# A chunked linear-attention and two-MLP kernel: one mask copied by another engine, two steps of round 2 put off, the waits of merged slots moved forward

## What is computed

```
for t in range(S):
    cur = np.einsum('bhd,bhe->bhde', u[None] * kt, vt)
    y[:, :, t] = np.einsum('bhd,bhde->bhe', rt, state + cur)
    state = wt[:, :, :, None] * state + np.einsum('bhd,bhe->bhde', kt, vt)
...
a = x @ w_a; b = x @ w_b                       # 384 x 1536
x = a * b @ w_out                              # 1536 x 384
h = x @ w_in                                   # 384 x 2048
g = np.maximum(h, 0.0) + alpha * np.minimum(h, 0.0)
out = g @ w_out                                # 2048 x 384
```

## Time and profile before

| | |
|---|---|
| median of 3 runs | 1011.1 us (1010.41 to 1011.45) |
| profiled execution, its time | 1010.97 us |
| its span, first to last instruction | 1009.2 us |
| mean granted TensorE clock | 0.998 |
| TensorE busy | 987.4 us (98%) |
| VectorE busy | 586.3 us (58%) |
| ScalarE busy | 296.8 us (29%) |
| GpSimd busy | 24.1 us (2%), all of it in the first 47 us |

### The profile page before, as it was taken

How to read it: one execution, slowest core, us unless ns; L and a number is a source line. 1 busy time by engine, 2 the same in 40 slices (tenths; PEclk the granted TensorE clock), 3 DMA queues, 4 the chain that set the end, 5 groups by cost and what they waited for, 6 DMA issues and landing times.

```text
span 1009.2 us, 26702 instructions
## 1 busy us (share of the span) xinstructions
PE 987.4 (98%) x11200; PEld 963.8 (96%) x11200; DVE 586.3 (58%) x1209; ACT 296.8 (29%) x628; POOL 24.1 (2%) x24
## 2 busy tenths in 40 slices
PE   5799999999999999999999999999999999999998
PEld 5799999999999999999999999999999999999998
DVE  7796765855857658567432437555555555555554
ACT  3435314223242242341223324222222222222212
POOL 4400000000000000000000000000000000000000
PEclk9999999999999999999999999999999999999999
DMA  6554311312113013110020414010101010101000
GB/s 174 144 149 121 93 38 34 111 30 65 53 29 92 25 36 87 53 37 2 25 60 15 128 32 126 8 40 11 38 13 35 13 34 14 32 16 32 20 6 23
DMA packets 42126, 52.88 MB, mean 52 GB/s; under 512 B 5152, under 2 KB 42016, under 8 KB 42016
## 3 DMA queue, kind: packets, MB, share of 16 engines
q1 hardware_dynamic: 40624, 51.04, 17.7%
q10 hardware_dynamic: 1392, 0.25, 0.2%
HBM read 39.48 MB, written 9.44 MB: 48 GB/s over the span
## 4 chain that ended last, share of the span: by engine, by line
PE 95%; DVE 3%; issue 1%; ACT 0%; ACTq 0%; DMA 0%; DVEq 0%; SPq 0%
PE products L170 18%; PE products L172 16%; PE products L171 16%; PE acc L170 12%; PE acc L171 12%; PE acc L172 12%; PE products L740 3%; PE products L758 1%; PE products L800 1%; PE products L816 1%; PE products L715 1%; PE products L785 1%; PE products L772 1%; DVE f_y L986 1%; DVE k_in L998 1%
## 5 line engine op out<-in xcount | busy, mean ns | idle before, releaser
L170 PE MATMUL products<-x_parts,weights_hi 128*128 128x384 f32 x576 | 202.2, 351 | 2.6 <-DMA x_parts<-f_y 2.0
L172 PE MATMUL products<-x_parts,weights_lo 128*128 128x384 f32 x576 | 195.1, 339 | 0.3 <-issue 0.3
L171 PE MATMUL products<-x_parts,weights_hi 128*128 128x384 f32 x576 | 194.7, 338 | 0.0
L1375 DVE TENSOR_SCALAR leaky_low<-products,leaky_al 128x384 f32<-128x384 f32 x128 | 79.1, 618 | 169.9 <-PE products L172 169.8
L1322 ACT ACTIVATE leaky_g_hi<-leaky_g_sb 128x384 fp32r<-128x384 f32 x128 | 67.3, 526 | 295.5 <-DVE leaky_g_sb L1380 183.8
L1235 DVE TENSOR_TENSOR g_sb<-a_g,products 128x384 f32<-128x384 f32 x96 | 53.1, 553 | 158.9 <-issue 90.8
L549 ACT ACTIVATE g_hi<-g_sb 128x384 fp32r<-128x384 f32 x96 | 50.3, 524 | 254.5 <-DVE g_sb L1235 254.5
L170 PEld LDWEIGHTS products<-x_parts,weights_hi 128*128 128x128 f32 x576 | 108.0, 187 | 7.8 <-issue 2.7
L172 PEld LDWEIGHTS products<-x_parts,weights_lo 128*128 128x128 f32 x576 | 108.2, 188 | 0.7 <-issue 0.7
L171 PEld LDWEIGHTS products<-x_parts,weights_hi 128*128 128x128 f32 x576 | 108.2, 188 | 0.0
L170 PE MATMUL acc<-g_hi,weights_hi 128*128 128x384 f32 x288 | 96.6, 336 | 0.0
(11 more groups left out here) (94 smaller groups left out, 1757.4 us busy)
## 6 DMA issues: line engine op xcount, KB each, us to landing
k_in<-in_k_dram SPq DMA_DIRECT2D x16, 336.0 KB, 3.9
r_in<-in_r_dram SPq DMA_DIRECT2D x16, 336.0 KB, 5.2
stage<-in_w_out_dram SPq DMA_DIRECT2D x14, 384.0 KB, 3.3
w_v<-in_v_dram SPq DMA_DIRECT2D x16, 288.0 KB, 3.6
y_dram<-x_in SPq DMA_DIRECT2D x8, 576.0 KB, 4.6
x_in<-y_dram SPq DMA_DIRECT2D x8, 576.0 KB, 4.6
out_dram<-leaky_out_sb SPq DMA_DIRECT2D x7, 576.0 KB, 3.3
stage<-in_w_dram SPq DMA_DIRECT2D x10, 336.0 KB, 3.8
```

What stands on the lines that cost most here:

```text
L170: pe.matmul(out, w_hi, x_hi, start=first, stop=False)
L171: pe.matmul(out, w_hi, x_lo, start=False, stop=False)
L172: return pe.matmul(out, w_lo, x_hi, start=False, stop=last)
L1375: dve.tensor_scalar(self.low[f % 2][:, :], h, 0.0, self.al[:, f:f + 1], ALU.min, ALU.mult).then_inc(self.low_ready, 1)
```

## The change

Three things. `copy_four_mask` goes from VectorE (phase 7 of round 0) to ScalarE, behind its preparation of k and r, ahead of the first split of weights. In round 2 the first steps of stream 1 leave phase 0: that of r (`step_r(n, 1, 0)`) comes at the end of phase 1, that of k (`first_step_k(n, 1)`) in phase 2 between the merge of stream 0 and the planes of stream 1. And the five waits of a merged slot stand ahead of the last third of `up_b` of the same block, in all of rounds 2 to 7, in phases 2 and 3; ahead of the slot only the wait for `g_ready` stays.

```diff
+                def copy_four_mask():
+
+                    act.wait_ge(masks_loaded, 32)
+                    dims = [2 * FOUR, Q // (2 * FOUR)]
+                    copy(view(four_mask, 0, [dims, [FOUR, 2], [1, FOUR]], P),
+                         view(level_mask, 0, [dims, [0, 2], [1, FOUR]], P)).then_inc(four_mask_ready, 1)
...
                 act.dma_start(ident[:, :], constants[0:ROWS, 0:ROWS]).then_inc(ident_loaded, 16)
+                copy_four_mask()
                 for step in range(BEFORE_TILES):
...
-                def four(n, j, g):
+                def wait_four(n, j):
 
                     pe.wait_ge(merged, merges(n, 0, 3))
                     pe.wait_ge(fours_merged, fours(n, j))
                     pe.wait_ge(k_first[j], n + 1)
                     pe.wait_ge(fours_copied[j], fours_round(n))
                     pe.wait_ge(fours_stepped[j], 2 * fours_round(n))
+
+                def four(n, j, g):
+
...
                         if kt == KT - 1 and f == F1 - 1 and tile < TILES - 1:
                             for block in range(KT):
                                 wait_x(tile + 1, block)
+                        if kt == KT - 1 and step_at(g) is not None:
+                            n, phase = divmod(step_at(g), PHASES)
+                            if n >= FOURS_FROM and phase in (2, 3):
+                                wait_four(n, phase - 2)
                         product = up_part(g, "w_b", b_ps(g), kt)
...
-                def first_steps(n):
-
-                    for j in range(2):
-                        first_step_k(n, j)
-                        step_r(n, j, 0)
+                def first_steps(n, j):
+
+                    first_step_k(n, j)
+                    step_r(n, j, 0)
...
                         if n == 2:
-                            first_steps(n)
+                            first_steps(n, 0)
...
                         if n == 1:
-                            first_steps(n)
+                            first_steps(n, 0)
+                            first_steps(n, 1)
                         products_of_w(n, 0, 2 if n < FOURS_FROM else 1, range(1, 7))
                         if n >= FOURS_FROM:
                             prepare_fours(n, 0)
+                        if n == 2:
+                            step_r(n, 1, 0)
                     elif phase == 2 and n >= FOURS_FROM:
                         merge_fours(n, 0)
+                        if n == 2:
+                            first_step_k(n, 1)
                         prepare_fours(n, 1)
...
-                    elif phase == 7 and n == 0:
-                        copy_four_mask()
-                    elif phase == 7:
+                    elif phase == 7 and n > 0:
```

More of the change, by code:

```diff
@@ L1021, in merge_level @@
                                         view(products, level_bank(phase, 0), [[BANK, 2], [32, 2 * CH], [h, 32 // h], [1, h]], P)).then_inc(merged, 2)
[L1023 to L1028, removed]
                 def prepare_fours(n, j):
```

## The result

The changed kernel took 1027.5 us, median of 5 (1026.3 to 1028.4), beside 1011.1 us before: 1.0161 times as long, 95% interval 1.0146 to 1.0176. Slower by 16.4 us, on the side that was forecast, and outside the range of 1020.0 to 1024.2.

The account below looks back on a forecast made before the run. It took TensorE, holding 95% of the chain, as the bound. Mask -2.0, round 2 +1.6 and rounds 3 to 7 +11.3 summed to +10.9 on 1010.97, the median 0.1 above: 1022.0 us, range 1020.0 to 1024.2.

Parts of the forecast that it names:

- The waits moved forward, rounds 3 to 7: Phase 2, stream 1: TensorE stalls 2.25 us for VectorE's scratch product ahead of 12 wide products; five rounds, +11.3 us.
- Round 2: Phase 2 of round 2: the moved wait stalls TensorE, slot at 122.99 for 121.42, +1.6 us; postponed steps cost nothing.
- The mask: Kernel start: copy on ScalarE lets state sums start 1.8 us earlier and the first wide product 2.0 earlier: -2.0 us.
- the idle time would now be 1.4, so I expect no fall, and the narrow products behind it take about half: Kernel start, ahead of the weighted values: TensorE idle 1.4 us for 3.2, clock not falling to 0.50 as before.
- the transfers' issue: Kernel start: SyncE's loads until 38.26 let the last stores start at 38.3 to 38.4, 2.0 us earlier and no more.
- the clock falls in each stall: Rival, rounds 2 to 7: low clock costs 1.7 us behind each of six stalls, 10 us in all, 1032 us; 5%.
- the clock term: Behind the six stalls of rounds 2 to 7: the forecast's own case had no clock fall there, so no cost.

Follow-up runs that it names:

- e7: The changed kernel with phase 2's waits ahead of the first of the three blocks of down products: 1021.1 us, ratio 1.0095.
- e8: The changed kernel with phase 2's waits ahead of the third of the three blocks of down products: 1013.6 us, ratio 1.0023.
- e11: The changed kernel, with VectorE making stream 0's planes behind the first of six decay products, not behind the sixth: 1015.6 us, ratio 1.0045.
- e2: The kernel before with only round 2's two first steps put off, all waits at the slot: 1010.8 us, ratio 1.000.
- e9: e4 plus 16 products of the identity into a free bank ahead of the first wide product: 1011.3 us, ratio 1.0004.
- e1: The changed kernel with waits at the slot and round 2's steps as before, so only the mask's copy on ScalarE: 1009.3 us, ratio 0.9986.
- e6: The changed kernel plus 12 repeated wide products a round in phase 2 of rounds 2 to 7, filling TensorE's idle time: 1022.7 us, ratio 1.0109.
- e12: e4 plus the edits of e9 and e11 and nine products of zeros at the start: 1012.0 us, ratio 1.0012.
- e13: e4 plus e11's edit (stream 0's planes earlier, all waits at the slot): 1009.4 us, ratio 0.9986.
- e3: The kernel before with only the five waits moved forward, in phases 2 and 3: 1029.5 us, ratio 1.0174.
- e4: The changed kernel with the waits back at the slot in both phases, mask and steps kept: 1010.2 us, ratio 0.9994.

## Why the prediction was wrong, and where it was right

*The waits moved forward, rounds 3 to 7: right.* +2.25 a round was forecast, 2.26 is measured (11.3 in all), at the place, with the releaser and by the steps named, and e7, e8 and e11 move it as the sum says. By the Trainium skill's rule that matmuls keep program order the ready down products could not fill the stall, and they did not.

*Round 2: right.* 1.6 forecast, 1.57 without the clock. The postponed steps hurt nobody (e2).

*The mask: place right, size wrong.* The step that failed is "the idle time would now be 1.4, so I expect no fall, and the narrow products behind it take about half". They did not speed up: the 48 that start at 33.36 took 1.53, for 1.25 before. The view of stretches prints 1.00 before the clock's first change; the pace of the products says otherwise. 96 of the same kind take 2.17 at 29.70 and, in the kernel before, 1.29 at the full clock:

```profile
157.90 1.29 PE L785 MATMUL products<-w_v,scratch 64*48 64x48 f32 x96
```

And in e9, where the level rose at 32.4, the same 48 took 0.89 in place of 1.53:

```profile
34.29 0.89 PE L812 MATMUL products<-a_sb,w_v 64*48 64x64 f32 x48 [1.64 <-DVE state L1106]
```

So TensorE ran at the low level until the first change on record: until 37.1 in the changed kernel, and until 32.0 before, where the level rose while it was idle and fell again at 35.5. The end was not the transfers' issue but TensorE's own work: the store that is waited for was issued at 39.71 for 41.16, 1.45 earlier, and took 0.23 longer to land. That makes 1.22 us and not 2.0, and a fall behind the new first wide product took it back in that execution (e1 shows that it is not so in all).

*The clock behind the stalls: the step that put the time out of the range.* The prediction gave "the clock falls in each stall" 5%, and argued "the pause before 43.99 was 1.9 and the clock stayed at 1.00; the new ones are 2.1". One pause without a fall was taken as proof for six of nearly its length. In place of none or six there were three falls, at 1.55 each rather than 1.7: 4.65 us. With them and a mask term near zero the sum is 1010.97 + 12.9 + 4.65 = 1028.5, for 1028.09 in the profiled execution. Without them it is 1023.9, inside the range even with nothing from the mask; so it is the clock term, put at nothing, that failed. (The range's upper end adds up to 1024.1, not 1024.2.) The Trainium skill's warning (TensorE: Matmul & The Clock Gate, "Why this matters for your kernels") starts at gaps of about 3 us; here the clock fell behind idle stretches of 2.07, and the measurement decides. Which of six equal stalls has a fall behind it no run here tells; it is not their length. Behind the six pauses of 1.56 us of e7 its profile has none, but at the start of e1 the clock fell behind a pause of 1.75, so length alone does not decide it there either.

## What to carry to other kernels

Before a wait is moved forward in an engine's queue, take from the trace when its last semaphore comes and compare that with the new place, for each slot by itself: three products forward was free in phase 3, twelve cost 2.25 us a round in phase 2, because the order of the work around the slot is another there. A stall on TensorE can cost more than its length, since the clock can fall behind it: here behind three of six of 2.07 us, in each of two kernels. If it must be, useful or even useless products in it are cheaper than idleness (e6), but only as many as the stretch surely holds (e12). And where a slot is set by another engine, move that engine's work up first (e11, e13), the wait after.

## What the runs showed of the hardware that I had not expected

The mask's copy on VectorE does not have one price. In e3 it took 1.04 us, and 4.61 in the kernel before, with GpSimd's instructions at the same places within 0.03 us:

```profile
28.03 1.04 DVE L1034 COPY four_mask<-level_mask 128x32 f32<-128x32 f32 x1
30.94 0.26 DVE L1098 COPY state<-products 112x96 f32<-112x96 f32 x1 [1.87 <-PE products L788]
```

It ended there between GpSimd's step of r and its splits; in the kernel before, and in e2 (4.61 too), it missed that moment and the next. On ScalarE it takes 0.22. The Trainium skill, SBUF — State Buffer, "Who interferes with whom", says that whoever issues first keeps the shared ports for its whole instruction; who gets them when GpSimd's instructions follow one another closely differed here from profile to profile. That this makes the spread of the kernel before (1007.8 to 1013.2 us over the runs beside e1 to e4) is not shown: e4, with the copy on ScalarE, spreads as widely (1007.7 to 1012.6).

A wide product at the low level starts 0.32 us behind the one before, for 0.175 at the full one: 1.8 times, not twice.
